# Attention, MLP and a routed expert layer on one core: high halves of the expert weights on ScalarE, another order at the chunk seams

## The chip, the core and the metric

One NeuronCore of a Trainium2 chip runs the whole program. The time is the device time of one execution in microseconds. Five engines run their own instruction lists and meet in semaphores: TensorE (PE), VectorE (DVE), ScalarE (ACT), GpSimd (POOL) and SyncE (SP), which issues most DMAs. An instruction list is worked off in order: a wait in it holds all that stands behind it.

## What is computed

Three layers follow each other. B=4, heads H=8, sequence 576, head width 64, so 2304 tokens of 512 values.

```python
scores = scale * q @ k.T            # causal window of 64
x = softmax(masked scores) @ v      # -> (2304, 512)
h = x @ w_in                        # 512 x 2048
x = (h * sigmoid(1.702 * h)) @ w_out
noisy = x @ w_gate + log1p(exp(x @ w_noise)) * noise   # 8 experts
top2, weights = two largest of noisy, softmax over the two
out[t] = sum over the two of weight * relu(x[t] @ w1[e]) @ w2[e]   # 512 x 1024 x 512
```

## The kernel before

**Products in halves.** Matrices are multiplied as a high part (fp32r, a rounded copy) and a low part (value minus high): each product is three matmuls, high x high, low x high, high x low. So every operand is split by a copy and a subtraction.

**Stages.** Attention runs first. Then the MLP takes NG=6 chunks of TG=384 tokens. A chunk splits its x (split_x: four copies on ScalarE, four subtractions on VectorE), then runs FC=16 iterations c; n = 16g + c counts over all chunks. TensorE's `up` makes a 128-wide slice of h into one of two PSUM banks (12 matmuls), ScalarE makes the sigmoid, VectorE the product `gate`, ScalarE its high part (high_of_gate), VectorE its low part (low_of_gate), TensorE's `down` multiplies the slice with w_out into three y banks (9 matmuls). In order, ScalarE does sigmoid(n), then high_of_gate(n-1); TensorE does up(n), then down(n-2), at c=0 and c=1 too, where the down belongs to the chunk before.

**Routing of chunk g-1 inside chunk g.** copy_y takes the y banks to x2 at c=2; TensorE transposes x2 (turn_x2, from c=4), ScalarE copies the result, TensorE makes logits (from c=6), ScalarE and VectorE soften, choose, assign, weigh and place (c=9 to 14), ranks stands at c=13. Then POOL's scatter_x2(g-1) sends the rows to their experts' regions in DRAM by six indirect DMAs. copy_y of the next chunk waits until they have landed. After the last chunk the routing runs alone, then the routing tables are made (L1007 to L1037) and the experts begin.

**Expert weights.** While the MLP runs, 128 jobs of 256 KB split w1 and w2: SyncE loads raw data into one of four buffers (ej_loaded), POOL multiplies by one into `high` (L530, 3 buffers in xT, one extra) and subtracts (L532), SyncE stores both to split_weights. SyncE's order is load n, store n-2, load n+1, store n-1 and so on; load n waits for the stores of job n-4 to have landed. POOL does 8 jobs, then 24 jobs and a scatter, five times. Ahead of the first load SyncE writes zeros to all of `out` (6 DMAs of 768 KB) and to the pads of the experts' regions.

**Experts.** 40 tiles of 128 rows are used here, of at most SLOTS=43. For each tile, POOL gathers the rows of `out` so far (gather_part), VectorE adds the weighted result (finish, y_sb), and POOL scatters them back (scatter_y). A gather waits only for scatters of earlier experts (the table `settled`) and for its buffer. From tile j = SURE-1 = 35 on, POOL also waits for each scatter to have landed before it goes on (last lines of its block).

Of the kernel before, what the change touches and what calls it, by code (L numbers as in the profile page):

```python
# [11 lines left out]
P = 128  # L12
# [28 lines left out]
QUADS = 2  # L41
GQUADS = (EJOBS // 2 - QUADS) // (NG - 1)
# [9 lines left out]
FAR = 1 << 16  # L52
LG = 2 * E


def after(eng, sem, value):

    if isinstance(value, int) and value <= 0:
        return
    eng.wait_ge(sem, value)  # L60


def build(nc, q, k, v, w_in, w_out, w_gate, w_noise, noise, w1, w2, out):
# [13 lines left out]
    with ctx:  # L77
# [73 lines left out]
        count_to = sbc("count_to", [P, SLOTS])  # L151
        slot_row = sbc("slot_row", [P, SLOTS])
        upto = sbc("upto", [P, E, E], mybir.dt.bfloat16)
        odd = sbc("odd", [P, SLOTS + 1])
# [11 lines left out]
        expert_of = sbc("expert_of", [P, SLOTS], I32)  # L166
        row_of = sbc("row_of", [P, SLOTS], I32)
        ends = sbc("ends", [P, E], I32)
        rows = sbc("rows", [P, SLOTS], I32)
        slot_w = sbc("slot_w", [P, SLOTS])  # L170
        keep = sbc("keep", [P, SLOTS], I32)
        far = sbc("far", [P, SLOTS], I32)
        masked_id = sbc("masked_id", [P, SLOTS], I32)
        passed = sbc("passed", [P, SLOTS, E])
        stepped = sbc("stepped", [P, SLOTS, E])
        past = sbc("past", [P, SLOTS])
        row_f = sbc("row_f", [P, SLOTS])
        first_row = sbc("first_row", [P, SLOTS])
        first_slot = sbc("first_slot", [P, SLOTS])
        settled = sbc("settled", [P, SLOTS], I32)  # L180
        end_row = sbc("end_row", [P, SLOTS])
        valid = sbc("valid", [P, SLOTS])
# [294 lines left out]
        def _(pool):  # L477
# [97 lines left out]
            nc.gpsimd.iota(count_to[:], [[1, SLOTS]], base=0, channel_multiplier=0, allow_small_or_imprecise_dtypes=True).then_inc(slot_consts, 1)  # L575
            nc.gpsimd.iota(slot_row[:], [[P, SLOTS]], base=P, channel_multiplier=0, allow_small_or_imprecise_dtypes=True).then_inc(slot_consts, 1)
            nc.gpsimd.iota(odd[:].rearrange("p (a b) -> p a b", b=2), [[0, (SLOTS + 1) // 2], [1, 2]], base=0, channel_multiplier=0, allow_small_or_imprecise_dtypes=True).then_inc(slot_consts, 1)
# [50 lines left out]
            for j in range(SURE - 1, SLOTS):  # L628
                par = j % 2
                if j < SURE:  # L630
                    gather_part(j, par)
                    scatter_y(j, par)
                    for i in range(2):
                        pool.wait_ge(y_scattered[i], SURE // 2 * 16)
                else:
                    with pool.If(tiles1 > j + 1):
                        gather_part(j, par)
                        scatter_y(j, par)

                        pool.wait_ge(y_scattered[par], (j // 2 + 1) * 16)  # L640

        @block.scalar
        def _(act):
# [70 lines left out]

            def soften(g):
# [11 lines left out]
            def mlp(g, first):  # L727
                split_x(g)
                for c in range(FC):
                    n = g * FC + c  # L730
                    if c == 2 and not first:
# [15 lines left out]
                    if c == 12 and not first:  # L747
# [80 lines left out]
        def _(dve):  # L828
# [140 lines left out]
            def mlp(g, first):  # L969
                split_x(g)  # L970
                if g == 1:
# [47 lines left out]
            then(nc.vector.tensor_tensor(passed[:], end_e[:, None, :].to_broadcast([P, SLOTS, E]),  # L1019
                                         count_to[:, :, None].to_broadcast([P, SLOTS, E]), ALU.is_le))  # L1020
# [352 lines left out]
```

## Time and profile before

| | us |
|---|---|
| median of 3 runs | 1127.85 (1118.88, 1127.85, 1129.74) |
| profiled execution | 1117.89, its span 1116.2 |
| TensorE busy in the span | 998.9 (89%) |
| POOL, VectorE, ScalarE busy | 528.3, 628.7, 448.6 |
| TensorE's mean granted clock | 0.958 |

The profile is of one execution. Idle time of an engine is put down to what released it. The granted clock is a share of full speed: 1.0 is 2.4 GHz and 0.5 is 1.2 GHz. Attention lasts to about 164 us, the MLP from 164 to 598, the last routing to 642, the experts from there to the end.

### The profile page before, as it was taken

What the parts mean: (1) busy time and instruction counts of PE and PEld (TensorE: products, weight loads), DVE (VectorE), ACT (ScalarE), POOL (GpSimd) and SP (SyncE); (2) the same over time, 40 slices, a digit from 0 to 9 for tenths busy, and PEclk for the clock granted to TensorE, in tenths of its full rate; (3) what the DMA queues carried; (4) which work ended last, traced back from release to release, by engine and by line L of the source; (5) the groups of instructions that cost most, each with busy time, mean ns of one, the idle gap of its engine ahead of it and who ended that gap; (6) DMA issues with size and microseconds to landing.
All of it is one profiled execution on the core that took longest, in us unless ns stands there. A gap on an engine that the chain in (4) does not pass through costs nothing.

```text
span 1116.2 us, 21003 instructions
## 1 busy us (share of the span) xinstructions
PE 998.9 (89%) x5376; PEld 851.4 (76%) x5377; DVE 628.7 (56%) x1413; ACT 448.6 (40%) x1088; POOL 528.3 (47%) x511
## 2 busy tenths in 40 slices
PE   5777769999999999999996099999999999999993
PEld 5666659879899898898995078888887888888882
DVE  3777752342433527437353467676767676767671
ACT  4877762222424324233242034343443434343440
POOL 3555553896198889898985202121212121212121
PEclk8999989999999999999997599999999999999997
DMA  7678748998189799898888884586858585859211
GB/s 159 166 186 188 184 118 299 289 292 265 40 262 284 253 287 292 270 295 287 265 269 290 279 260 141 183 252 179 255 168 252 169 258 170 266 166 268 65 58 33
DMA packets 253444, 241.65 MB, mean 216 GB/s; under 512 B 97740, under 2 KB 171468, under 8 KB 253392
## 3 DMA queue, kind: packets, MB, share of 16 engines
q1 hardware_dynamic: 215312, 201.54, 60.4%
q0 software_dynamic: 9280, 28.62, 7.2%
q10 hardware_dynamic: 28800, 10.83, 4.3%
q8 instruction: 29, 0.48, 0.2%
q14 instruction: 23, 0.19, 0.1%
HBM read 148.81 MB, written 94.21 MB: 218 GB/s over the span
## 4 chain that ended last, share of the span: by engine, by line
PE 33%; DMA 17%; issue 13%; DVE 11%; ACT 9%; POOL 7%; ACTq 5%; DVEq 2%; POOLq 1%; SPq 1%
PE bank L1209 14%; PE bank L1224 13%; DMA part<-out,yrow 10%; ACT hq L783 4%; DMA out<-y_sb,yrow 4%; ACTq L766 3%; POOL raw L532 2%; ACT he L790 2%; POOL xT L530 2%; DVE y_sb L1079 2%; DMA w_raw<-moe_w_out 1%; PE bank L1244 1%; DVE hT L1067 1%; PE bank L1146 1%; DVEq L1041 1%
## 5 line engine op out<-in xcount | busy, mean ns | idle before, releaser
L1308 PE MATMUL bank<-W,xe 128*128 x960 | 233.2, 399 | 23.5 <-DVE xe L1054 23.5
L1319 PE MATMUL bank<-W,he 128*128 x960 | 230.5, 395 | 4.1 <-DVE he L1071 4.1
L1308 PEld LDWEIGHTS bank<-W,xe 128*128 128x128 f32 x960 | 182.1, 190 | 67.9 <-issue 23.6
L1209 PE MATMUL bank<-xs,W 128*128 128x384 f32 x1152 | 219.8, 340 | 8.7 <-DVE xs L895 8.6
L1224 PE MATMUL bank<-W,gs 128*128 128x512 f32 x864 | 217.1, 396 | 1.0 <-DVE gs L900 1.0
L1319 PEld LDWEIGHTS bank<-W,he 128*128 128x128 f32 x960 | 179.9, 188 | 49.0 <-issue 5.8
L1209 PEld LDWEIGHTS bank<-xs,W 128*128 128x128 f32 x1152 | 200.3, 189 | 17.0 <-issue 10.3
L1224 PEld LDWEIGHTS bank<-W,gs 128*128 128x128 f32 x864 | 161.7, 188 | 31.9 <-DVE gs L900 1.4
L982 DVE TENSOR_TENSOR gate<-bank,gate 128x384 f32<-128x384 f32 x96 | 53.4, 557 | 232.6 <-ACT gate L736 226.2
L606 POOL DMA_INDIRECT out<-y_sb,yrow x40 | 40.6, 1015 | 291.5 <-DVE y_sb L1079 286.1
L783 ACT ACTIVATE hq<-bank 32x256 f32<-32x256 f32 x320 | 119.7, 374 | 112.7 <-issue 99.9
L736 ACT ACTIVATE gate<-bank 128x384 f32<-128x384 f32 x96 | 47.2, 492 | 281.6 <-PE bank L1209 275.0
L1065 DVE STREAM_TRANSPOSE hT<-bank 32x256 f32<-32x256 f32 x320 | 144.0, 450 | 11.2 <-PE bank L1308 6.2
L532 POOL TENSOR_TENSOR raw<-raw,xT 128x512 fp32r<-128x512 f32 x96 | 129.7, 1351 | 7.5
L530 POOL TENSOR_TENSOR xT<-raw,e_iota 128x512 fp32r<-128x512 f32 x96 | 107.0, 1115 | 38.4 <-DMA raw<-moe_w 37.1
L900 DVE TENSOR_TENSOR gs<-gate,gs 128x384 fp32r<-128x384 f32 x96 | 85.1, 888 | 0.0
L773 ACT ACTIVATE xe<-xr 128x512 fp32r<-128x512 f32 x40 | 25.3, 632 | 139.4 <-DVE xr L1050 136.7
L509 POOL TENSOR_TENSOR prob<-prob,rden 128x384 f32<-128x384 f32 x48 | 39.8, 829 | 74.2 <-DVE rden L852 74.2
L1071 DVE SCALAR_TENSOR_TENSOR he<-hT,he 128x1024 fp32r<-128x1024 f32 x40 | 49.0, 1226 | 45.1 <-ACT he L790 45.1
L661 ACT ACTIVATE prob<-prob,nmx 128x128 f32<-128x128 f32 x144 | 56.1, 391 | 27.8 <-DVE nmx L845 27.6
L560 POOL DMA_INDIRECT x_by_expert<-x,xT x36 | 36.9, 1024 | 58.0 <-issue 37.5
L599 POOL DMA_INDIRECT part<-out,yrow x40 | 42.0, 1050 | 34.9 <-POOL yrow L596 34.9
(148 smaller groups left out, 1031.8 us busy)
## 6 DMA issues: line engine op xcount, KB each, us to landing
W<-split_weights SPq DMA_DIRECT2D x128, 512.0 KB
raw<-moe_w SPq DMA_DIRECT2D x128, 256.0 KB, 3.4
split_weights<-raw SPq DMA_DIRECT2D x128, 256.0 KB, 3.3
split_weights<-xT SPq DMA_DIRECT2D x96, 256.0 KB, 3.1
xg<-x_by_expert ACTq DMA_DIRECT2D x160, 64.0 KB
split_weights<-high SPq DMA_DIRECT2D x32, 256.0 KB
q_raw<-q SPq DMA_DIRECT2D x32, 144.0 KB, 2.9
k_raw<-k SPq DMA_DIRECT2D x32, 144.0 KB, 3.9
```

What stands on the lines that cost most here:

```text
L530: nc.gpsimd.tensor_tensor(high[buf], job_raw[buf], one, ALU.mult).then_inc(ej_high, 1)
L532: nc.gpsimd.tensor_tensor(job_raw[buf].bitcast(F32R), job_raw[buf], high[buf].bitcast(F32), ALU.subtract).then_inc(ej_low, 1)
L661: ins = nc.scalar.activation(prob[m % 3][:, b], prob[m % 3][:, b], ACT.Exp, bias=nmx[:, m % 2, b:b + 1], accum_out=den[:, m % 2, b:b + 1])
L783: ins = nc.scalar.activation(hq[c * Q:(c + 1) * Q, :].rearrange("p (k q i) -> p k q i", q=2, i=Q)[:, :, q], src[q * Q:(q + 1) * Q, :, c], ...
L900: nc.vector.tensor_tensor(gs[c % 2][:, 1], gate[c % 2][:], gs[c % 2][:, 0].bitcast(F32), ALU.subtract).then_inc(g_low, 1)
L982: nc.vector.tensor_tensor(gate[c % 2][:], h_ps[c % 2][:, 0:TG], gate[c % 2][:], ALU.mult).then_inc(gated, 1)
L1065: nc.vector.transpose(dst[c * Q:(c + 1) * Q, :, q], src[q * Q:(q + 1) * Q, :, c])
L1071: nc.vector.scalar_tensor_tensor(out=he[par][:, 1], in0=hT[:], scalar=0.0, in1=he[par][:, 0].bitcast(F32), op0=ALU.max, op1=ALU.subtract). ...
L1209: ins = nc.tensor.matmul(h_ps[c % 2][:, 0:TG], w_in_s[:, wl, d, c * P:(c + 1) * P], xs[:, xl, d], start=(d == 0 and wl + xl == 0), stop=(d ...
L1224: ins = nc.tensor.matmul(y_ps[t][:], gs[c % 2][:, gl, t * P:(t + 1) * P], w_out_s[:, wl, c], start=(c == 0 and gl + wl == 0), stop=(c == F ...
L1308: ins = nc.tensor.matmul(h2_ps[par][:, f * 512:(f + 1) * 512], xe[par][:, xl, d * P:(d + 1) * P], weights(e, wl, d * FE + f * 512), start= ...
L1319: ins = nc.tensor.matmul(ye_ps[par][:], he[par][:, hl, c * P:(c + 1) * P], weights(e, wl, W1COLS + c * DM), start=(c == 0 and wl + hl == 0 ...
```

## The change

- POOL only subtracts (low_of_job). The high parts are copies on ScalarE (high_of_job), put into its MLP iterations by the formula jobs_by: 128 jobs over n=1 to n=93, one or two in each. They stand after high_of_gate and wait for ej_loaded there. c=0 has two from the second chunk on, c=8 two.
- scatter_x2(g) stands on POOL behind the subtractions of the jobs up to c=13 of chunk g+1.
- At a seam TensorE does down(14), up(0), down(15); c=1 has only its up; from c=2 up(c), down(c-2) as before. ScalarE and VectorE finish gate 15 ahead of c=0; high_of_gate(0) comes in c=1, behind copy_y and sigmoid(1).
- copy_y moves from c=2 to c=1, and all of the routing two iterations ahead; place is at c=12.
- The tables get two more columns (TABLE = SLOTS+2); the waits on each scatter at the tail go, and one wait for all scatters stands at the end, its counts read from `settled`.
- SyncE's list is unchanged.

```diff
+def jobs_by(chunk):
+    return min(JOBS, max(0, (chunk - 1) * JOBS // (NG * FC - 3)))
...
-            def split_job(n, buf, count):
-                pool.wait_ge(ej_loaded[buf], count * 16 + 16)
-                one = e_iota[:, None, 1:2].to_broadcast([P, DC, P])
-                nc.gpsimd.tensor_tensor(high[buf], job_raw[buf], one, ALU.mult).then_inc(ej_high, 1)
+            def low_of_job(n):
+                buf = n % 4
                 pool.wait_ge(ej_high, n + 1)
                 nc.gpsimd.tensor_tensor(job_raw[buf].bitcast(F32R), job_raw[buf], high[buf].bitcast(F32), ALU.subtract).then_inc(ej_low, 1)
...
-            pool.wait_ge(xs_low, DC)
-            for i in range(QUADS):
-                for buf in range(4):
-                    split_job(i * 4 + buf, buf, i)
-            for g in range(1, NG):
-                with pool.Fori(QUADS + (g - 1) * GQUADS, QUADS + g * GQUADS) as i:
-                    for buf in range(4):
-                        split_job(i * 4 + buf, buf, i)
-                scatter_x2(g - 1)
+            done = 0
+            for g in range(NG - 1):
+                due = jobs_by((g + 1) * FC + 14)
+                for n in range(done, due):
+                    low_of_job(n)
+                done = due
+                scatter_x2(g)
+            for n in range(done, JOBS):
+                low_of_job(n)
...
                 if j < SURE:
                     gather_part(j, par)
                     scatter_y(j, par)
-                    for i in range(2):
-                        pool.wait_ge(y_scattered[i], SURE // 2 * 16)
                 else:
                     with pool.If(tiles1 > j + 1):
                         gather_part(j, par)
                         scatter_y(j, par)
-                        pool.wait_ge(y_scattered[par], (j // 2 + 1) * 16)
+            for i in range(2):
+                written = pool.value_load(settled[0:1, SLOTS + i:SLOTS + i + 1], min_val=SURE // 2 * 16, max_val=SLOTS * 16)
+                pool.wait_ge(y_scattered[i], written)
+                pool.sem_inc(wait_passed, 1)
...
+            def high_of_job(n):
+                buf = n % 4
+                act.wait_ge(ej_loaded[buf], n // 4 * 16 + 16)
+                nc.scalar.activation(high[buf], job_raw[buf], ACT.Copy).then_inc(ej_high, 1)
...
             def mlp(g, first):
                 split_x(g)
+                if not first:
+                    high_of_gate(g * FC - 1, FC - 1)
                 for c in range(FC):
                     n = g * FC + c
-                    if c == 2 and not first:
+                    if c == 1 and not first:
                         copy_y(g - 1, 0)
                         copy_y(g - 1, 2)
                     act.wait_ge(hidden, n + 1)
                     after(act, g_low, n - 1)
                     nc.scalar.activation(gate[c % 2][:], h_ps[c % 2][:, 0:TG], ACT.Sigmoid, scale=1.702).then_inc(sigmoided, 1)
-                    if not (first and c == 0):
-                        high_of_gate(n - 1, (c - 1) % FC)
-                    if 5 <= c < 5 + GT and not first:
-                        if c == 5:
+                    if c:
+                        high_of_gate(n - 1, c - 1)
+                    for job in range(jobs_by(n), jobs_by(n + 1)):
+                        if job == 0:
+                            act.wait_ge(xs_low, DC)
+                        high_of_job(job)
+                    if 3 <= c < 3 + GT and not first:
+                        if c == 3:
                             act.wait_ge(out_zeroed, ZEROED)
-                        copy_x2T(g - 1, c - 5)
-                    if c == 10 and not first:
+                        copy_x2T(g - 1, c - 3)
+                    if c == 8 and not first:
                         nc.scalar.preload_act_table_set("natural_log_exp_and_others")
                         soften(g - 1)
                         nc.scalar.preload_act_table(ACT.Sigmoid)
-                    if c == 12 and not first:
+                    if c == 10 and not first:
...
             def mlp(g, first):
                 split_x(g)
+                if not first:
+                    low_of_gate(g * FC - 1, FC - 1)
...
                 for c in range(FC):
                     n = g * FC + c
-                    if c == 2 and not first:
+                    if c == 1 and not first:
                         copy_y(g - 1)
                     dve.wait_ge(sigmoided, n + 1)
                     nc.vector.tensor_tensor(gate[c % 2][:], h_ps[c % 2][:, 0:TG], gate[c % 2][:], ALU.mult).then_inc(gated, 1)
-                    if not (first and c == 0):
-                        low_of_gate(n - 1, (c - 1) % FC)
+                    if c:
+                        low_of_gate(n - 1, c - 1)
                     if not first:
+                        if c == 7:
+                            soften(g - 1)
                         if c == 9:
-                            soften(g - 1)
+                            choose(g - 1)
+                        if c == 10:
+                            assign(g - 1)
                         if c == 11:
-                            choose(g - 1)
+                            weigh(g - 1)
                         if c == 12:
-                            assign(g - 1)
-                        if c == 13:
-                            weigh(g - 1)
-                        if c == 14:
                             place(g - 1)
...
             def mlp(g, first):
                 for c in range(FC):
                     n = g * FC + c
+                    if c == 0 and not first:
+                        down(n - 2, FC - 2, g - 1)
                     up(g, c, n)
-                    if not (first and c < 2):
-                        down(n - 2, (c - 2) % FC, g if c >= 2 else g - 1)
+                    if c == 0 and not first:
+                        down(n - 1, FC - 1, g - 1)
+                    if c >= 2:
+                        down(n - 2, c - 2, g)
                     if not first:
+                        if 2 <= c < 2 + GT:
+                            turn_x2(g - 1, c - 2)
                         if 4 <= c < 4 + GT:
-                            turn_x2(g - 1, c - 4)
-                        if 6 <= c < 6 + GT:
-                            logits(g - 1, c - 6)
-                        if c == 13:
+                            logits(g - 1, c - 4)
+                        if c == 11:
                             ranks(g - 1)
```

## Rows read from the trace of the kernel before

**Rows 1.** The windows view: stretch, its length, busy us by engine, PEclk, DMA share, GB/s.

```profile
174.00:180.00 6.00, 6.00 (x31) 5.37 (x30) 1.62 (x4) 1.81 (x4) 0.00 (x0) 1.00 1.03 384
...
232.00:234.00 2.00, 1.78 (x6) 1.67 (x6) 0.24 (x2) 0.40 (x2) 1.92 (x2) 0.50 0.69 216
...
322.00:400.00 78.00, 77.06 (x408) 69.27 (x407) 34.63 (x72) 26.43 (x53) 68.72 (x58) 1.00 0.88 278
```

**Rows 2.** The page's parts 5 and 6: busy, mean ns, idle before; DMA to landing.

```profile
L1209 PE MATMUL bank<-xs,W 128*128 128x384 f32 x1152 | 219.8, 340 | 8.7 <-DVE xs L895 8.6
...
L532 POOL TENSOR_TENSOR raw<-raw,xT 128x512 fp32r<-128x512 f32 x96 | 129.7, 1351 | 7.5
...
L773 ACT ACTIVATE xe<-xr 128x512 fp32r<-128x512 f32 x40 | 25.3, 632 | 139.4 <-DVE xr L1050 136.7
...
raw<-moe_w SPq DMA_DIRECT2D x128, 256.0 KB, 3.4
```

**Rows 3.** The groups view by line: a table load of ScalarE.

```profile
L744 ACT ACT_TABLE_LOAD x4 | 5.1, 1283 | 0.1
```

**Rows 4.** The timeline, start of the MLP: start us, us, engine, line, operation, idle before.

```profile
163.99 6.49 PE L1209 MATMUL bank<-xs,W 128*128 128x384 f32 x36 [1.70 <-DVE xs L895]
...
168.43 0.49 ACT L736 ACTIVATE gate<-bank 128x384 f32<-128x384 f32 x1 [1.59 <-PE bank L1209]
...
170.32 2.26 PE L1224 MATMUL bank<-W,gs 128*128 128x512 f32 x9
...
173.23 9.77 SPq L410 DMA_DIRECT2D raw<-moe_w  x3
...
174.50 2.26 PE L1224 MATMUL bank<-W,gs 128*128 128x512 f32 x9
...
185.87 1.04 POOL L530 TENSOR_TENSOR xT<-raw,e_iota 128x512 fp32r<-128x512 f32 x1 [21.87 <-DMA raw<-moe_w]
```

**Rows 5.** The timeline, TensorE at the seam of chunks 0 and 1.

```profile
228.99 1.28 PE L1209 MATMUL bank<-xs,W 128*128 128x384 f32 x6 [2.08 <-DVE xs L895]
...
233.36 2.61 PE L1224 MATMUL bank<-W,gs 128*128 128x512 f32 x9
```

**Rows 6.** The timeline, first jobs after a scatter: a store, later a load.

```profile
310.62 0.56 SPq L415 DMA_DIRECT2D split_weights<-xT  x1
...
314.92 0.35 SPq L410 DMA_DIRECT2D raw<-moe_w  x1
...
318.82 1.04 POOL L530 TENSOR_TENSOR xT<-raw,e_iota 128x512 fp32r<-128x512 f32 x1 [0.74 <-DMA raw<-moe_w]
...
531.33 0.56 SPq L415 DMA_DIRECT2D split_weights<-xT  x1
...
536.41 0.35 SPq L410 DMA_DIRECT2D raw<-moe_w  x1
```

**Rows 7.** The timeline: a turn inside the MLP, then the end of the MLP.

```profile
546.78 0.60 PE L1237 MATMUL bank<-ident,x 128*128 128x128 f32 x4
...
593.49 4.46 PE L1224 MATMUL bank<-W,gs 128*128 128x512 f32 x18 [0.99 <-DVE gs L900]
...
594.74 1.15 POOL L560 DMA_INDIRECT x_by_expert<-x,xT  x1 [0.15 <-issue]
...
607.76 1.97 PE L1237 MATMUL bank<-ident,x 128*128 128x128 f32 x8 [9.82 <-ACT x L707]
```

**Rows 8.** The chain that ended last: the last scatter's landing.

```profile
601.31 5.42 DMA x_by_expert<-x,xT
```

**Rows 9.** The timeline, the last tiles.

```profile
1092.64 5.87 PE L1319 MATMUL bank<-W,he 128*128 x24 [1.57 <-DVE he L1071]
...
1094.86 1.02 POOL L606 DMA_INDIRECT out<-y_sb,yrow  x1 [5.36 <-issue]
...
1099.85 0.18 POOL L596 COPY yrow<-rows 128x1 int32<-128x1 int32 x1 [3.97 <-issue]
...
1104.40 0.75 DVE L1079 SCALAR_TENSOR_TENSOR y_sb<-bank,slot_w,part 128x512 f32<-128x512 f32 x1 [11.33 <-DMA part<-out,yrow]
```

More of the change, by code:

```diff
@@ L40 @@
 KEPT = 2
-QUADS = 2
-GQUADS = (EJOBS // 2 - QUADS) // (NG - 1)
+JOBS = 2 * EJOBS
 SLOTS = (N * KEPT + E * (P - 1) + E - 1) // P
@@ L52 @@
 FAR = 1 << 16
+TABLE = SLOTS + 2
 LG = 2 * E
@@ L150, in build @@
         to_consts = sbc("to_consts", [P, 2 * TG])
-        count_to = sbc("count_to", [P, SLOTS])
-        slot_row = sbc("slot_row", [P, SLOTS])
+        count_to = sbc("count_to", [P, TABLE])
+        slot_row = sbc("slot_row", [P, TABLE])
         upto = sbc("upto", [P, E, E], mybir.dt.bfloat16)
-        odd = sbc("odd", [P, SLOTS + 1])
+        odd = sbc("odd", [P, TABLE + 1])
         lane = sbc("lane", [P, 1])
@@ L165, in build @@
         hT = sbc("hT", [P, FE])
-        expert_of = sbc("expert_of", [P, SLOTS], I32)
-        row_of = sbc("row_of", [P, SLOTS], I32)
+        expert_of = sbc("expert_of", [P, TABLE], I32)
+        row_of = sbc("row_of", [P, TABLE], I32)
         ends = sbc("ends", [P, E], I32)
[L169 to L182, printed above, removed]
+        rows = sbc("rows", [P, TABLE], I32)
+        slot_w = sbc("slot_w", [P, TABLE])
+        keep = sbc("keep", [P, TABLE], I32)
+        far = sbc("far", [P, TABLE], I32)
+        masked_id = sbc("masked_id", [P, TABLE], I32)
+        passed = sbc("passed", [P, TABLE, E])
+        stepped = sbc("stepped", [P, TABLE, E])
+        past = sbc("past", [P, TABLE])
+        row_f = sbc("row_f", [P, TABLE])
+        first_row = sbc("first_row", [P, TABLE])
+        first_slot = sbc("first_slot", [P, TABLE])
+        settled = sbc("settled", [P, TABLE], I32)
+        end_row = sbc("end_row", [P, TABLE])
+        valid = sbc("valid", [P, TABLE])
         arenas = [[xT[:, d, TG:2 * TG], TG, 0] for d in range(2)]
@@ L562, in scatter_x2 @@
                                                 bounds_check=last_x, oob_is_err=False).then_inc(x2_scattered, 16)
[L564 to L572 removed]
+            done = 0
[7 more added lines that the diff above has]
+                low_of_job(n)
             pool.wait_ge(xs_low, NG * DC)
[L575 to L577 removed]
+            nc.gpsimd.iota(count_to[:], [[1, TABLE]], base=0, channel_multiplier=0, allow_small_or_imprecise_dtypes=True).then_inc(slot_consts, 1)
+            nc.gpsimd.iota(slot_row[:], [[P, TABLE]], base=P, channel_multiplier=0, allow_small_or_imprecise_dtypes=True).then_inc(slot_consts, 1)
+            nc.gpsimd.iota(odd[:].rearrange("p (a b) -> p a b", b=2), [[0, (TABLE + 1) // 2], [1, 2]], base=0, channel_multiplier=0, allow_small_or_imprecise_dtypes=True).then_inc(slot_consts, 1)
             nc.gpsimd.iota(lane[:], [[0, 1]], base=0, channel_multiplier=1, allow_small_or_imprecise_dtypes=True).then_inc(slot_consts, 1)
@@ L1018, in _ @@
             nc.vector.tensor_scalar_add(ends[:], end_e, 1.0)
-            then(nc.vector.tensor_tensor(passed[:], end_e[:, None, :].to_broadcast([P, SLOTS, E]),
-                                         count_to[:, :, None].to_broadcast([P, SLOTS, E]), ALU.is_le))
+            then(nc.vector.tensor_tensor(passed[:], end_e[:, None, :].to_broadcast([P, TABLE, E]),
+                                         count_to[:, :, None].to_broadcast([P, TABLE, E]), ALU.is_le))
             then(nc.vector.reduce_sum(past[:], passed[:], AX.X))
             nc.vector.tensor_single_scalar(expert_of[:], past[:], float(E - 1), ALU.min)
-            then(nc.vector.tensor_tensor(stepped[:], passed[:], tiles_e[:, None, :].to_broadcast([P, SLOTS, E]), ALU.mult))
+            then(nc.vector.tensor_tensor(stepped[:], passed[:], tiles_e[:, None, :].to_broadcast([P, TABLE, E]), ALU.mult))
             nc.vector.scalar_tensor_tensor(out=first_row[:], in0=past[:], scalar=float(CAP), in1=slot_row[:], op0=ALU.mult, op1=ALU.add)
             then(nc.vector.reduce_sum(first_slot[:], stepped[:], AX.X))
-            then(nc.vector.tensor_tensor(settled[:], first_slot[:], odd[:, 0:SLOTS], ALU.add))
+            then(nc.vector.tensor_tensor(settled[:], first_slot[:], odd[:, 0:TABLE], ALU.add))
             then(nc.vector.tensor_single_scalar(settled[:], settled[:], 1, ALU.arith_shift_right))
@@ L1029, in _ @@
             then(nc.vector.scalar_tensor_tensor(out=first_row[:], in0=first_slot[:], scalar=-float(P), in1=first_row[:], op0=ALU.mult, op1=ALU.add))
-            then(nc.vector.tensor_tensor(stepped[:], passed[:], end_step[:, None, :].to_broadcast([P, SLOTS, E]), ALU.mult))
+            then(nc.vector.tensor_tensor(stepped[:], passed[:], end_step[:, None, :].to_broadcast([P, TABLE, E]), ALU.mult))
             then(nc.vector.reduce_sum(end_row[:], stepped[:], AX.X))
```

## The prediction

> **What bounds the kernel now.** I read the busy time by stretch first, then the groups by line, then the timeline at the four places where the first layer's weights, its chunk seams, the hand-over to the experts and the last tile lie. In the middle of the MLP TensorE is busy 77.06 of 78 us [rows 1], so there only what holds TensorE counts. One iteration c is an up and a down: the downs of c=2 and c=3 start at 170.32 and 174.50, 4.18 us apart, 2.09 for each half [rows 4]. ScalarE and VectorE have slack: the down that needs a sigmoid starts 1.9 us after that sigmoid did (168.43 to 170.32) [rows 4], and TensorE gets to it 4.2 us after the sigmoid's up has ended. A sigmoid can be late by about 4.2 - 0.2 - 1.9 = 2.1 us at no cost.
>
> TensorE loses time in three places. At the chunk seams up(0) waits for the split of x: L1209 has 8.7 us of such idle time [rows 2], 1.7 of it at the very start [rows 4], so 7.0 at seams; at the first seam the idle of 2.08 us [rows 5] is followed by a granted clock of 0.50, which is the 1.2 GHz level [rows 1]. That up, begun at 228.99, is followed by its down at 233.36: 4.37 us, less the 2.09 of a normal up and 0.63 of further idle, leaves 1.65, and the down takes 0.35 longer: 2.0 us for the low clock. At the end of the MLP there is 0.99 us, and then 9.82 us until the first transpose [rows 7], because copy_y needs scatter_x2(4) landed, and that stood behind 24 split jobs on POOL. Last, at the tail the gather for tile 39 waits for the scatter of tile 38 [rows 9].
>
> **Gains.** (a) With down(14) ahead of up(0), the split of x has 2.09 us more; the largest first wait was 2.08. All 7.0 + 2.0 go, and the 0.99 too, since POOL's subtractions end at c=13: 10.0 us.
>
> (b) Hand-over. Count from the end of up(13) of the last chunk. ScalarE does sigmoid, gate copy and two jobs (0.2 + 0.9 + 2 x 0.63, [rows 2]) until 2.4; POOL subtracts (1.35 each, [rows 2]) until about 4.4; the six indirect DMAs start 6.6 us from first to last (594.74 to 601.31, [rows 7, 8]), and the last needs 5.42 to land [rows 8]: 16.4, or 15.6 if POOL is not behind with a job. TensorE ends its last down at 2 x 4.18 + 3 x 2.09 = 14.6. The first transpose starts 1.0 after the landing (606.73 to 607.76, [rows 7, 8]). Idle 2.0 to 2.8 in place of 9.82, so 7.4 gained (7.0 to 7.9). Eight transposes took 1.97 there [rows 7], four take 0.60 at full clock [rows 7]; with less idle ahead the clock may hold for this part: 1.0 taken, 0 to 2.5 possible. Together 8.4.
>
> (c) Tail. POOL issues scatter 38 at 1094.86, and copies yrow only at 1099.85 (3.97 us idle); y_sb of tile 39 starts at 1104.40 [rows 9]. Without the wait the copy can follow at once, or 1.05 us later for the register load; TensorE's last down, begun at 1092.64 and 5.87 long [rows 9], is ahead of that gather. 3.4 us (2.9 to 3.9). The final wait at the end moves nothing.
>
> The 128 high parts, 1.1 us each off POOL, were on no path of TensorE apart from (b).
>
> **Losses, first: job 0.** The new ScalarE program puts high_of_job(0) into n=1, with its wait on ej_loaded ahead of sigmoid(2). SyncE's order is not changed: the zeros for out and the pads go first, and in 174 to 180 the DMA share is 1.03 [rows 1]. The first raw loads are issued at 173.23 and job 0's data is there at 185.8: POOL waited 21.87 us for it and started at 185.87 [rows 4]. POOL could wait for free. ScalarE can't: its queue behind job 0 holds sigmoid(2), then high(1), and TensorE needs high(1) for down(1). So ScalarE copies until 186.5, sigmoid(2) starts at 186.55, down(1) at 188.45 instead of 174.50. That is 14.0 us of idle, and the restart is at the low clock, 2.0 us by the first seam. Loads 1 and 2 were issued in the same row and are in by then. 16.0 us; bounds 14 (clock held) to 18.
>
> **Second: the seam after each scatter.** Count from the end of up(14). POOL does low(38) (job numbers of the first such seam), then six indirect DMAs, from -1.0 to 6.7, during which nothing is subtracted. low(39) ends at 8.1 and low(40) at 9.5. SyncE issues load n, store n-2, load n+1, store n-1: so load 42 stands behind store 39 and goes out at 9.6, load 43 needs store 39 landed. After the scatters of before, a load waited for the store of the same buffer 4.3 us (310.62 to 314.92) and 5.1 us (531.33 to 536.41); the load issued at 314.92 was used at 318.82, after a wait: 3.9 [rows 6]; the median of all is 3.4 [rows 2]. So load 42 is in at 13.1 and load 43 at 8.2 + 5.0 + 3.4 = 16.6 (16.0 to 17.1). By the formula of jobs_by both fall into c=0 of the next chunk (31*128/93 = 42 for n=32, 32*128/93 = 44 for n=33; 22 more at each later seam), and ScalarE wants them at 11.2 and 11.8. Behind them in its queue: copy_y twice (1.1), sigmoid(1), high(0). Job 43's copy ends at 17.3, sigmoid(1) starts at 18.5, down(0) 1.9 later at 20.4. TensorE is at down(0) at 4.18 + 6 x 2.09 = 16.7: 3.7 us of idle (3.0 to 4.2), four times (the seams behind scatters 0 to 3). The nearest row for the clock is the first seam, where 2.7 us of idle within 5.3 cost 2.0: taken here too, between 0 and 2.0. Four times 5.7 = 22.8 (12 to 25).
>
> For a DMA of 256 KB there is another figure. The Trainium skill ("DMA: Bandwidth & Descriptors", Anatomy of one DMA) fits 2.0 us plus bytes over 436 GB/s, which is 2.6 us (an estimate by that page, and for the software path). The trace doesn't agree: its median for such a load is 3.4 [rows 2]. By that page, with 0.7 for the second store's issue, job 43 would be in at 14.1, the seam's stall would be 1.2 and the whole sum, with no clock loss, +0.5.
>
> **Third: c=8.** It holds two jobs (1.3 us) and soften with two table loads of 1.28 [rows 3] and two small activations, some 3.1. Sigmoid, gate copy and these end 5.5 after the up; the next sigmoid was due at 4.4, so it is 1.1 late, 1.7 with a short load wait: within the 2.1 of slack unless VectorE is slow as well. 0 to 1.8 per chunk; 0.3 taken, 1.5 in all.
>
> ScalarE's load is no bound: 1.84 us of each 4.18 in the mean. The DMA pace is none either: 0.77 MB per 3.04 us is 252 GB/s, and 278 were carried in 322 to 400 [rows 1]. The two wider columns of the tables and the longer straight-line programs are taken as 0.
>
> **Sum.** 16.0 + 22.8 + 1.5 - 10.0 - 8.4 - 3.4 = +18.5 us. Against the profiled execution (1117.89 us; span 1116.2) that is 1136.4. That execution is at the low end: the runs are 1118.88, 1127.85 and 1129.74. I put the sum on the middle of the four, 1123.6: **1142 us**, 1.6% more.
>
> **Rivals.** (1) Seams stall, but the clock holds: 3.7 us in one piece is less time than the 5.3 us over which the first seam's trouble was spread, with TensorE busy before and after. 4 x 2.0 less: +10.5, 1134. (2) ScalarE is late inside the chunk too: at c=8 the full 1.8 each time, 9 instead of 1.5. Speaks for it: two jobs and two table loads in one iteration. +26, 1150. (3) Short seams: a store is back as soon as the median load, 3.4, so that job 43 is in at 15.0; stall 2.1, no clock loss. Speaks for it: right after a scatter the DMA queues are empty. Against it: the 4.3 to 5.1 of [rows 6] were measured at just that point. 4 x 3.6 less: +4.1, 1128. (4) The other side, faster: ScalarE's waits on loads never reach TensorE, as the change needs. Place: ej_loaded in high_of_job; all losses but c=8 vanish, -20.3, 1103. It decides once TensorE's stalls by jobs stay under about 9 us in all; the start alone has 14 by [rows 4], so for this job 0's load would have to land by 173.
>
> **How the numbers follow.** About 1% is what a measurement of this kernel tells from no change, here 11 us. Forecast 0.42; clock holds at seams 0.20; c=8 0.13; short seams 0.15; never waits 0.10. Slower by over 1%: forecast, c=8 and half of the clock case, 0.65. Within 1%: short seams and the other half, 0.25. Faster: 0.10. The range leaves out the last case alone and part of its neighbours: from short seams with job 0's stall at its lower bound, on a low run (1118.9 + 2.1 = 1121), to c=8 on the high run (1129.7 + 26 = 1156). The likeliest case's own range is 1130 to 1150.
>
> **What the profile after would show.** Right: on ScalarE one wait for raw of some 16 us near 170, TensorE idle about 14 us from 174.5; at four seams TensorE idle 3 to 4 us ahead of down(0), put down to gs or ScalarE, with ScalarE waiting on raw before; no wait of up(0) for xs; idle before the first transpose at the hand-over 2 to 3 us; last y_sb 3.4 us sooner after the last down. Wrong: sigmoid(2) on time (then the losses are not there), or the seam waits gone although POOL scatters for 7.7 us, or waits of TensorE inside chunks, which would mean the pace of the loads bounds.

## The result, and the profile after

| | before | after |
|---|---|---|
| median, side by side on one chip (14 runs each) | 1123.78 us (1116.85 to 1129.74) | 1132.47 us (1129.36 to 1145.01) |
| profiled execution | 1117.89 | 1132.05, its span 1130.2 |
| TensorE busy | 998.9 | 1006.7 |
| POOL, VectorE, ScalarE busy | 528.3, 628.7, 448.6 | 378.3, 605.8, 517.3 |
| TensorE's mean granted clock | 0.958 | 0.953 |

The ratio is 1.009, 95% interval 1.0059 to 1.0121. The changed kernel is slower, by about one per cent. The rows below are of the kernel after unless a sentence says otherwise; L1225 is up, L1240 down, L909 VectorE's split of x, L914 its low_of_gate, L721 high_of_job, L534 low_of_job.

From the page's part 5, the groups (busy, mean ns | idle before, releaser):

```profile
L1240 PE MATMUL bank<-W,gs 128*128 128x512 f32 x864 | 221.1, 402 | 19.8 <-DVE gs L914 19.8
...
L1225 PE MATMUL bank<-xs,W 128*128 128x384 f32 x1152 | 221.2, 343 | 6.9 <-DVE xs L909 6.9
...
L998 DVE TENSOR_TENSOR gate<-bank,gate 128x384 f32<-128x384 f32 x96 | 53.6, 558 | 273.9 <-ACT gate L746 255.8
...
L914 DVE TENSOR_TENSOR gs<-gate,gs 128x384 fp32r<-128x384 f32 x96 | 60.0, 625 | 1.2 <-ACT gs L702 1.2
```

TensorE's idle time in the MLP is 26.7 us here (19.8 ahead of downs, 6.9 ahead of ups). Before, it was 9.7: 8.7 ahead of ups [rows 2] and 0.99 ahead of the last downs [rows 7]. The timeline shows where it lies. First the start of the MLP, ScalarE and TensorE (start us, us, engine, line, operation, idle before):

```profile
186.60 0.63 ACT L721 ACTIVATE xT<-raw 128x512 fp32r<-128x512 f32 x1 [14.22 <-DMA raw<-moe_w]
...
164.81 8.71 PE L1225 MATMUL bank<-xs,W 128*128 128x384 f32 x36 [1.70 <-DVE xs L909]
...
189.05 4.21 PE L1240 MATMUL bank<-W,gs 128*128 128x512 f32 x9 [11.35 <-DVE gs L914]
...
195.36 2.26 PE L1240 MATMUL bank<-W,gs 128*128 128x512 f32 x9
```

ScalarE waits for job 0's raw data until 186.60, and down(1) starts at 189.05, 24.24 us after the MLP's first up, where it was 10.51 in [rows 4]: 13.7 later. The next down follows after 6.31 instead of 4.18, which is 2.1 of low clock (granted 0.50 in the window of 189 to 193). That is 15.9 us.

Then the four seams behind a scatter, TensorE:

```profile
319.35 3.76 PE L1225 MATMUL bank<-xs,W 128*128 128x384 f32 x12 [2.58 <-DVE xs L909]
...
394.34 3.72 PE L1240 MATMUL bank<-W,gs 128*128 128x512 f32 x9 [4.21 <-DVE gs L914]
...
471.89 2.32 PE L1225 MATMUL bank<-xs,W 128*128 128x384 f32 x12 [2.58 <-DVE xs L909]
...
545.32 3.81 PE L1240 MATMUL bank<-W,gs 128*128 128x512 f32 x9 [4.22 <-DVE gs L914]
```

The idle time is 2.58 + 4.21 + 2.58 + 4.22 = 13.6 us. At three of the four the group behind it takes 3.7 to 3.8 us instead of 2.25: the low clock. At the first, the next up starts at 325.17, 1.64 us later than two normal halves of 2.09 behind 319.35 would put it; three times that is 4.9. In all 18.5 us. The windows view of 319 to 323 has the clock at 0.60, against 1.00 just ahead:

```profile
315.00:319.00 4.00, 1.77 (x8) 1.11 (x6) 4.00 (x1) 1.11 (x3) 3.77 (x4) 1.00 0.60 208
319.00:323.00 4.00, 3.65 (x13) 3.69 (x14) 2.08 (x5) 0.00 (x0) 0.00 (x0) 0.60 0.98 294
```

The waits of 2.58 us stand ahead of up(0). Those of 4.21 and 4.22 us stand ahead of down(14), which comes before up(0) in the new order.

**What holds TensorE there is VectorE, and what holds VectorE goes with POOL.** VectorE and POOL at the first two of these seams:

```profile
314.49 6.12 DVE L909 TENSOR_TENSOR xs<-xT,xs 128x384 fp32r<-128x384 f32 x4 [0.32 <-issue]
...
313.82 1.20 POOL L562 DMA_INDIRECT x_by_expert<-x,xT  x1 [0.30 <-issue]
315.02 1.32 POOL L534 TENSOR_TENSOR raw<-raw,high 128x512 fp32r<-128x512 f32 x1
316.28 2.50 POOL L534 TENSOR_TENSOR raw<-raw,xT 128x512 fp32r<-128x512 f32 x2
...
389.07 0.56 DVE L998 TENSOR_TENSOR gate<-bank,gate 128x384 f32<-128x384 f32 x1 [3.63 <-issue]
389.54 4.74 DVE L914 TENSOR_TENSOR gs<-gate,gs 128x384 fp32r<-128x384 f32 x1
...
390.14 2.50 POOL L534 TENSOR_TENSOR raw<-raw,xT 128x512 fp32r<-128x512 f32 x2
392.59 1.27 POOL L534 TENSOR_TENSOR raw<-raw,high 128x512 fp32r<-128x512 f32 x1
```

While POOL ran the indirect DMAs of the scatter, three jobs (39 to 41 at the first seam) piled up, and it subtracts them back to back: 315.02 to 318.78, and 390.14 to 393.86. The one subtraction of VectorE that meets this burst ends only 0.42 us after it, at 319.20 and 394.28. By the view of line L909, at the first seam that is one operation of 4714 ns among four whose median is 546. At the fourth seam low_of_gate begins only at 541.94, inside the burst of 541.11 to 544.84, lasts 3.33 us and again ends 0.43 us behind it. Whether it is the split of x or low_of_gate depends on which is due then. The product at L998, which reads one operand from PSUM, has the mean 558 ns (559 at most) against 557 before, when POOL was busier; the low part, with both operands in SBUF, went from 888 to 625.

In before, POOL's instructions never held VectorE that long although it had more of them: no operation of the split or of low_of_gate lasted over 1.65 us. POOL's subtraction waited for its own multiplication, and the trace has a break of 0.1 us between the two. VectorE at the seam of chunks 0 and 1, and POOL beside it, of before:

```profile
225.86 1.45 DVE L900 TENSOR_TENSOR gs<-gate,gs 128x384 fp32r<-128x384 f32 x1
227.23 4.95 DVE L895 TENSOR_TENSOR xs<-xT,xs 128x384 fp32r<-128x384 f32 x4
...
225.85 1.05 POOL L530 TENSOR_TENSOR high<-raw,e_iota 128x512 fp32r<-128x512 f32 x1
226.97 1.46 POOL L532 TENSOR_TENSOR raw<-raw,high 128x512 fp32r<-128x512 f32 x1
```

POOL is idle from 226.90 to 226.97. The low part at 225.86 ended at 227.31, 0.41 us behind POOL's multiplication, although POOL's next subtraction had begun: the break let it in. Of VectorE's four split operations behind it the longest took 1.63 us and the shortest 0.55 (the view of L895): none was held for more than about one instruction of POOL.

**The hand-over and the tail** gained what they should, nearly:

```profile
625.54 1.09 PE L1253 MATMUL bank<-ident,x 128*128 128x128 f32 x8 [3.24 <-ACT x L709]
...
1110.81 5.87 PE L1339 MATMUL bank<-W,he 128*128 x24 [1.56 <-DVE he L1087]
...
1113.02 1.02 POOL L608 DMA_INDIRECT out<-y_sb,yrow  x1 [8.35 <-issue]
1114.05 0.20 POOL L598 COPY yrow<-rows 128x1 int32<-128x1 int32 x1
...
1118.62 0.75 DVE L1095 SCALAR_TENSOR_TENSOR y_sb<-bank,slot_w,part 128x512 f32<-128x512 f32 x1 [7.39 <-issue]
```

The first transpose waits 3.24 us instead of 9.82 [rows 7]. The copy of yrow now follows the scatter at once, and y_sb starts 7.81 us after the last down instead of 11.76 [rows 9]; from that down to the span's end it is 19.39 instead of 23.56.

**The account, profile to profile:** attention +0.8, first up to last down +23.5, idle ahead of the transposes -6.6, last routing -0.2, experts +0.6, tail -4.2: +13.9 of the 14.0 us by which the span grew. In first up to last down, job 0 and the seams have +15.9 and +18.5, so some 10.9 us were gained there. The medians differ by only 8.7: the profiled execution of before lay 5.9 us under its own median, that of after 0.4 under its own. Which stage makes before's executions differ among themselves is not known.

### The profile page after: what moved, and what is told of

The parts are those of the page before. It is cut to its first block, busy times and chain, and to the rows that moved or that the text cites. A ratio compares the mean times of both kernels' runs of the same rounds, so it can differ in the third digit from the quotient of the medians.

```text
span 1130.2 us, 20791 instructions
## 1 busy us (share of the span) xinstructions
PE 1006.7 (89%) x5376; PEld 858.6 (76%) x5377; DVE 605.8 (54%) x1413; ACT 517.3 (46%) x1216; POOL 378.3 (33%) x383
## 4 chain that ended last, share of the span: by engine, by line
PE 62%; DMA 9%; issue 8%; DVE 7%; ACT 6%; POOL 2%; ACTq 2%; SPq 1%; DVEq 1%; POOLq 0%
PE bank L1225 16%; PE bank L1240 15%; PE bank L1339 13%; PE bank L1328 13%; DMA part<-out,yrow 3%; ACT hq L797 2%; PE bank L1260 2%; DMA out<-y_sb,yrow 1%; PE bank L1162 1%; ACTq L780 1%; DMA w_raw<-moe_w_in 1%; DMA w_raw<-moe_w_out 1%; DMA raw<-moe_w 1%; DMA x_by_expert<-x,xT 1%; DVE gs L914 1%
## 5 line engine op out<-in xcount | busy, mean ns | idle before, releaser
L1240 PE MATMUL bank<-W,gs 128*128 128x512 f32 x864 | 221.1, 402 | 19.8 <-DVE gs L914 19.8
L1225 PE MATMUL bank<-xs,W 128*128 128x384 f32 x1152 | 221.2, 343 | 6.9 <-DVE xs L909 6.9
L1225 PEld LDWEIGHTS bank<-xs,W 128*128 128x128 f32 x1152 | 204.0, 192 | 13.1 <-issue 7.8
L1240 PEld LDWEIGHTS bank<-W,gs 128*128 128x128 f32 x864 | 164.6, 192 | 52.6 <-DVE gs L914 21.0
L998 DVE TENSOR_TENSOR gate<-bank,gate 128x384 f32<-128x384 f32 x96 | 53.6, 558 | 273.9 <-ACT gate L746 255.8
L534 POOL TENSOR_TENSOR raw<-raw,xT 128x512 fp32r<-128x512 f32 x96 | 123.1, 1290 | 202.7 <-ACT xT L721 202.6
L1081 DVE STREAM_TRANSPOSE hT<-bank 32x256 f32<-32x256 f32 x320 | 144.0, 450 | 10.9 <-PE bank L1328 5.9
L721 ACT ACTIVATE xT<-raw 128x512 fp32r<-128x512 f32 x96 | 58.5, 623 | 18.2 <-DMA raw<-moe_w 18.2
L914 DVE TENSOR_TENSOR gs<-gate,gs 128x384 fp32r<-128x384 f32 x96 | 60.0, 625 | 1.2 <-ACT gs L702 1.2
L534 POOL TENSOR_TENSOR raw<-raw,high 128x512 fp32r<-128x512 f32 x32 | 41.3, 1291 | 49.4 <-ACT high L721 49.4
L804 ACT ACTIVATE he<-hT 128x1024 fp32r<-128x1024 f32 x40 | 42.5, 1061 | 33.6 <-DVE hT L1083 32.1
```

The lines of the kernel that those rows point to most:

```text
L721: nc.scalar.activation(high[buf], job_raw[buf], ACT.Copy).then_inc(ej_high, 1)
L914: nc.vector.tensor_tensor(gs[c % 2][:, 1], gate[c % 2][:], gs[c % 2][:, 0].bitcast(F32), ALU.subtract).then_inc(g_low, 1)
L998: nc.vector.tensor_tensor(gate[c % 2][:], h_ps[c % 2][:, 0:TG], gate[c % 2][:], ALU.mult).then_inc(gated, 1)
L1081: nc.vector.transpose(dst[c * Q:(c + 1) * Q, :, q], src[q * Q:(q + 1) * Q, :, c])
L1225: ins = nc.tensor.matmul(h_ps[c % 2][:, 0:TG], w_in_s[:, wl, d, c * P:(c + 1) * P], xs[:, xl, d], start=(d == 0 and wl + xl == 0), stop=(d ...
L1240: ins = nc.tensor.matmul(y_ps[t][:], gs[c % 2][:, gl, t * P:(t + 1) * P], w_out_s[:, wl, c], start=(c == 0 and gl + wl == 0), stop=(c == F ...
```

## Experiments

Every run was timed against before on the same chip; ratios are to before, with their 95% intervals. Edits are on the changed kernel unless said. Idle times are those of each kernel's profiled execution.

**late: the jobs begin at n=6 instead of n=1.** It tests the start term.

```diff
-    return min(JOBS, max(0, (chunk - 1) * JOBS // (NG * FC - 3)))
+    return min(JOBS, max(0, (chunk - 6) * JOBS // (NG * FC - 8)))
```

> The changed kernel, with the 128 jobs given out over n=6 to n=93 in place of n=1 to n=93; nothing else moves. Theory: ScalarE's wait for job 0 holds TensorE at the start of the MLP, and that costs about 13.7 us of delay of down(1) plus 2.1 us of low clock after it; then TensorE has no idle time above 1 us in the first chunk and the time falls by 14 to 16 us against the changed kernel (about 1117, ratio to before 0.994 to 0.997). Rival: the first loads are late whatever ScalarE does, or the denser later jobs (one more in every 20 iterations) make new waits in the chunks: then 8 us or less are won.

Measured 1117.39 us, ratio 0.9967 (0.9941 to 0.9992). No idle time is left in the first chunk but the 1.70 us at its start; the seams stay (2.58, 4.06, 2.60, 2.58 us). From 1.009 to 0.9967 is 13.8 us, for a term of 15.9 in the trace. The 4.06 has another wait in it: the jobs now stand closer together, and ScalarE waited 2.84 us for raw data, until 379.71, just ahead of its copies for the split.

**c0shift: no job in c=0.** From the second chunk on, c=0 to 5 get 0, 1, 2, 2, 2, 1 jobs in place of 2, 1, 1, 2, 1, 1. If ScalarE's wait for load 43 made the stall, as predicted, it goes.

```diff
-                    for job in range(jobs_by(n), jobs_by(n + 1)):
+                    jobs = range(jobs_by(n), jobs_by(n + 1))
+                    if not first and c < 6:
+                        lo = jobs_by(g * FC)
+                        jobs = range(lo + (0, 0, 1, 3, 5, 7)[c], lo + (0, 1, 3, 5, 7, 8)[c])
+                    for job in jobs:
```

> The changed kernel, with the two jobs of c=0 moved behind c=1 and c=2 in chunks 1 to 5 (0, 1, 2, 2, 2, 1 jobs in c=0 to 5). Theory of the prediction (ScalarE waits at c=0 for load 43, which stands behind the scatter): the seam idle of TensorE, 2.6, 4.2, 2.6, 4.2 us in the trace after, goes, and the time falls by 13 us or more. Rival (VectorE's subtraction at the seam is held by the three subtractions that POOL does back to back after a scatter, 6.1 us for four split operations or 4.7 us for one of the gate): the seam idle stays at 2.6 to 4.2, the time moves by less than 2 us.

Measured 1128.79 us, ratio 1.0081 (1.0053 to 1.0109): nothing gained that stands out of the noise. All four seams of this kernel have 2.57 or 2.58 us ahead of up(0); the first and the last:

```profile
313.78 3.54 PE L1229 MATMUL bank<-xs,W 128*128 128x384 f32 x12 [2.57 <-DVE xs L913]
...
540.14 3.74 PE L1229 MATMUL bank<-xs,W 128*128 128x384 f32 x12 [2.58 <-DVE xs L913]
```

**lowwait: POOL waits, behind the scatter, for the split of x before its backlog.** It takes the overlap of POOL and VectorE away.

```diff
                 scatter_x2(g)
+                if g < NG - 2:
+                    pool.wait_ge(xs_low, (g + 3) * DC)
```

> The changed kernel, with one wait added on POOL: after each scatter (not the last) the subtractions go on only when the next chunk's x is split. Rival theory (VectorE held by POOL): VectorE's four split operations take 2.0 us in all and no gate subtraction above 1.4 us at seams; up(0) does not wait for xs; but the loads 42 and 43 come about 2 us later, so that ScalarE waits on raw in c=0 and down(0) is 2 to 4 us late at four seams. Time against the changed kernel within 4 us. Theory of the prediction alone (loads bound the seam, VectorE does not): seam idle grows by 2 us each, 8 us slower or more.

Measured 1130.08 us, ratio 1.0089 (1.0059 to 1.0119). The wait for xs is gone and another stands in its place. TensorE, then ScalarE, of this kernel at the first such seam:

```profile
326.24 2.94 PE L1242 MATMUL bank<-W,gs 128*128 128x512 f32 x9 [2.68 <-DVE gs L916]
...
320.94 0.63 ACT L723 ACTIVATE xT<-raw 128x512 fp32r<-128x512 f32 x1 [3.10 <-DMA raw<-moe_w]
323.15 0.63 ACT L723 ACTIVATE high<-raw 128x512 fp32r<-128x512 f32 x1 [1.58 <-DMA raw<-moe_w]
```

The four are 2.68, 3.40, 2.69 and 3.80 us, ahead of down(0), with ScalarE waiting on raw in c=0: the stall that had been predicted, in its place. But the edit makes a part of it. POOL now stands still ahead of its backlog at each of the four seams, and the stores and loads behind it come later by as much:

```profile
314.98 1.53 POOL L534 TENSOR_TENSOR raw<-raw,high 128x512 fp32r<-128x512 f32 x1 [1.52 <-DVE xs L911]
```

Less these 1.5 us, an estimate for the stall by the loads alone is 1.2, 1.9, 1.2 and 2.3 us, where 3.7 each had been predicted.

**both: c0shift and lowwait together.**

> The last two together: no jobs at c=0, and POOL's subtractions after a scatter wait for the split of x. If VectorE held by POOL is the first limit of the seam and the load of job 43 the second, only the two together clear it: seam idle under 1 us each, no low clock there, 15 to 18 us less than the changed kernel. If one of the two edits alone already gives that, the other theory falls. If a third limit is there, the seam idle stays above 1 us.

Measured 1111.14 us, ratio 0.9909 (0.9884 to 0.9934). No seam has any idle time. Either edit alone gave 1 us or nothing, the two give 1.009 - 0.9909 = 0.0181, 20.3 us, beside the 18.5 counted in the trace. Two limits lay one behind the other: VectorE held by POOL, and, once POOL waits, ScalarE behind the loads.

**gap: behind each of the three backlog subtractions POOL sets a small spare tile to zero** (the line that allocates it is left out here). Does an instruction that reads nothing let VectorE in?

```diff
                     low_of_job(n)
+                    if g and n - done < 3:
+                        nc.gpsimd.memset(spare[:, (g - 1) * 3 + n - done], 0.0)
```

> The changed kernel, with a memset of 12 columns on POOL behind each of the three subtractions that follow a scatter. It reads nothing. Theory A: VectorE's subtraction gets its turn only when POOL has a moment without a reading instruction, and in a burst there is none; with the memsets one of VectorE's operations is held by one subtraction (1.3 us), not by three (3.9 to 4.2 us), so the longest split operation falls below 2 us and seam idle drops to 2 us or less. Theory B: VectorE is held by POOL's queue as a whole, or waits for all of the burst for another reason (it has to be idle): no change, 3 to 4.7 us for the longest operation, seam idle 2.6 and 4.2 us as after.

Measured 1134.94 us (two runs), ratio 1.0116 (1.0078 to 1.0154). VectorE and POOL of this kernel:

```profile
313.26 4.90 DVE L917 TENSOR_TENSOR gs<-gate,gs 128x384 fp32r<-128x384 f32 x1
...
313.93 1.29 POOL L535 TENSOR_TENSOR raw<-raw,high 128x512 fp32r<-128x512 f32 x1
315.14 0.13 POOL L573 MEMSET spare<- 128x12 f32 x1
315.21 1.27 POOL L535 TENSOR_TENSOR raw<-raw,xT 128x512 fp32r<-128x512 f32 x1
```

No: the operation of VectorE is held over the whole burst, zeroing and all.

**drain: POOL waits for its own last subtraction before each of the three.** This puts back the break that before had.

```diff
                 for n in range(done, due):
+                    if g and n - done < 3:
+                        pool.wait_ge(ej_low, n)
                     low_of_job(n)
```

> Edit: on the changed kernel, POOL waits, before each of the three backlog subtractions behind a scatter, for the semaphore of its own subtraction before, so that one is complete before the next begins. Theory (the wait is VectorE's, held as long as POOL's subtractions follow one another without a break, and a break lets it in): no operation of VectorE with two inputs in SBUF at the four seams lasts over some 2 us, where 3.33 to 6.12 for one or four stood; TensorE's idle there falls from 2.58, 4.21, 2.58 and 4.22 us to under 1 each, about -10 us of idle and -4 of low clock, ratio 0.995 to 1.000 instead of 1.009. Rival (it is the sum of POOL's work that costs, or a break of this length is not seen by VectorE): the four waits stay within 0.5 us of 2.6 and 4.2 us and the ratio stays at 1.007 to 1.012. Second rival (with the first limit gone ScalarE's wait on the loads behind the scatter shows, as with the early wait on POOL): waits of 2 to 4 us on VectorE's low part of the gate's result, with ScalarE idle on raw before them, ratio 1.004 to 1.010.

Measured 1123.67 us, ratio 1.0011 (0.9989 to 1.0033), some 9 us better than the changed kernel. VectorE and POOL of this kernel at the first such seam:

```profile
315.24 5.85 DVE L911 TENSOR_TENSOR xs<-xT,xs 128x384 fp32r<-128x384 f32 x4 [0.32 <-ACT xs L699]
...
315.78 1.31 POOL L534 TENSOR_TENSOR raw<-raw,high 128x512 fp32r<-128x512 f32 x1
317.18 3.03 POOL L534 TENSOR_TENSOR raw<-raw,xT 128x512 fp32r<-128x512 f32 x2
```

From 317.09 to 317.18 POOL does nothing, and that is enough: the four operations of VectorE take 2283, 1631, 1623 and 545 ns instead of one 4714 and three of 546. The first ends at 317.52. The sum is nearly the same, but the first parts come early enough for up(0) to start, and TensorE's waits are 0.70 and 0.75 us at each seam (at the third 0.15 more), no longer 2.6 or 4.2. That is above the 1 us per seam that I expected, one operation lasts over 2 us, and the ratio lies just above the expected 0.995 to 1.000; direction and cause hold. The loads made no stall here: c=0 has its two jobs as in the changed kernel, and no down(0) waits at any of the four seams; ScalarE's own waits for raw data there are 0.73 and 0.65 us at the second and the fourth.

**late_c0_drain: late, c0shift and drain.**

> Edit: the jobs spread over the later part of the MLP, those of the chunks behind a scatter moved to the chunks after, and POOL waiting for its own last subtraction before each of the three of the backlog. Theory (breaks let VectorE in): no seam with over 1 us of idle, as with the early wait in POOL in place of the breaks, which gave 1104.0 us and ratio 0.983; expected 1101 to 1107 us, ratio 0.980 to 0.987. Rival (breaks do nothing): four waits of 2.6 us on VectorE's split as in the run that moved the jobs alone, some 10 to 14 us more, ratio 0.992 to 0.998.

Measured 1111.67 us, ratio 0.9917 (0.9888 to 0.9945). That lies between the two expectations. TensorE's waits at the seams are 1.46, 2.59, 1.65 and 1.45 us, so breaks do less than keeping POOL away. At the second seam a wait of ScalarE for raw data (2.11 us, to 376.18) ahead of the copies for the split has a part in it, as in late.

**late_both: late, c0shift and lowwait.** In this kernel and in late_c0_drain the last number of c0shift's table is `jobs_by(g * FC + 6) - lo` in place of 8, as late's formula gives 9 jobs in some chunks.

> The changed kernel with the three edits tried before: jobs over n=6 to n=93, none in c=0, POOL waits for the split of x behind a scatter. If the two causes (job 0's wait, the seam) are independent, their gains add: 14 us and 17 to 19 us off the changed kernel, about 1100, ratio to before 0.98. If the seam edit only worked because job 0's stall had shifted the work against the loads, less than 25 us in all.

Measured 1104.02 us, ratio 0.9829 (0.9795 to 0.9864): the lowest median of this study, ahead of both; its interval meets that of late_inter below. In the MLP only 1.70 us of idle remain beside the 1.70 at its start:

```profile
375.13 2.33 PE L1231 MATMUL bank<-xs,W 128*128 128x384 f32 x12 [1.70 <-DVE xs L915]
```

The two gains, 0.0123 and 0.0181, would give 0.9786 if they added in full; it is 0.0043 (4.8 us) short of that, which four ratios with intervals of 0.0025 to 0.0035 to either side do not tell from nothing. Against before it is 19.2 us faster, for gains of 21.8 (10.0 + 8.4 + 3.4) in the prediction.

**late_inter: late, and the backlog's three subtractions go one each between the last scatter DMAs.** Another way to break the burst.

```diff
-            def scatter_x2(g):
+            def scatter_x2(g, between=()):
...
+                        if between and at in between:
+                            for n in between[at]:
+                                low_of_job(n)
...
-                scatter_x2(g)
+                extra = range(due, min(JOBS, due + 3))
+                scatter_x2(g, {at: [n] for at, n in zip((3, 4, 5), extra)})
+                done = due + len(extra)
```

> Two edits on the changed kernel: jobs over n=6 to n=93, and on POOL the three subtractions that follow a scatter are put between its last three indirect DMAs, so no burst of three stands at the seam and the stores of those jobs go out up to 4 us earlier. Theory (VectorE held by the burst first, load of the second job of c=0 next): both causes shrink together, seam idle under 1 us at each of four seams, no wait for job 0. Time 1100 to 1106, ratio to before 0.98 to 0.985. Rival: a single subtraction on POOL is enough to hold the split of x, or the scatter gets so much longer that copy_y waits for it: seam idle of 1 to 2.5 us stays, 1108 to 1115.

Measured 1106.43 us, ratio 0.9865 (0.9841 to 0.9888), 0.0102 (11.4 us) under late, between the two times that were expected. The seams have 0.58, 2.83, 1.07 and 0.82 us where late has 11.8 in all. The 2.83 is not VectorE held by a burst: ScalarE waited 2.80 us for raw data, until 373.04, ahead of its copies for the split.

**tail: before, with the change's two table columns and its waits at the tail alone.** The lines that go are shown; the wider tables and the one wait at the end are as in the change:

```diff
-                    for i in range(2):
-                        pool.wait_ge(y_scattered[i], SURE // 2 * 16)
...
-                        pool.wait_ge(y_scattered[par], (j // 2 + 1) * 16)
```

> The kernel before with the tail's part of the change alone: the tables two columns wider, no waits on each scatter from tile 35 on, one wait at the end. Expected from the trace after (last down's start to the end 19.4 us against 23.6): 4 us faster, ratio 0.996, and y_sb of the last tile within 8 us of the last down's start. Rival: the gain in the trace after was an accident of that execution, or needs the routing's other timing: ratio 1.0.

Measured 1115.55 us, ratio 0.9947 (0.9917 to 0.9976), which is 3 to 9 us less. The trace has the last y_sb 7.9 us after the last down, as the changed kernel has it.

The hand-over was not tried alone: its gain is read from the trace.

## Why the prediction was right, and where it was not

It said 1142 us and slower; 1132.47 came, inside the range, and slower by 0.6 to 1.2%, at the edge of what the text called slower. The rise was 8.7 us where 18.5 had been added up. The start, the hand-over and the tail were right in mechanism. At the seams the mechanism was wrong, and that its size came near is luck.

- **Job 0: right.** Predicted 14.0 of idle and 2.0 of clock, measured 13.7 and 2.1. The first three ups happened to run at a lower clock (granted 0.71 in 165 to 173; 8.71 instead of 6.49 us), so only 11.35 of it shows as idle. late confirms it with 13.8.
- **Seams behind scatters: size near, cause wrong.** 22.8 us predicted, 18.5 measured. The failing step is "VectorE is ready, ScalarE waits for load 43". The count of POOL's work was right (six DMAs, then a backlog), but it was followed only through what waits for POOL's results, not through what runs beside them. The text's test "no wait of up(0) for xs" failed at two of four seams, and at the other two the wait was ahead of down(14); none was ahead of down(0). c0shift, alone, refutes the named cause. lowwait shows that it stood one step behind, at an estimated 1.2 to 2.3 us without that edit's own delay, for a predicted 3.7; drain, where up(0) is late by only some 1.5 us, shows no such stall at all. One input was mis-sized: the load of the same buffer went out 3.1 us after the first store at the seam (316.50 to 319.61), and 3.7, 3.1 and 3.7 at the others, not the 5.0 taken from the 4.3 and 5.1 of [rows 6]. With 3.1 and 3.7 the prediction's own chain gives a stall of 1.8 or 2.4.
- **Clock at the seams:** taken at 2.0 four times, it was about 1.6 three times. The rival in which the clock holds was wrong at three, right at one.
- **Seams before (a): right.** No idle time at the seam of chunks 0 and 1, none ahead of the last downs; "both" has none at any seam. 10.0 predicted, some 10.9 by the account above.
- **Hand-over (b):** 7.4 of idle predicted, 6.6 measured; of the 1.0 for the clock 0.2 came, since the routing behind took 34.8 us instead of 35.0.
- **Tail (c):** 3.4 predicted, 4.2 measured.
- **c=8:** 1.5 predicted, no idle time there. This rival is out, as is "never waits". (The pace of the loads in that section is 259 GB/s for 768 KB in 3.04 us, not 252; it stays below the 278 that it is compared with.)
- **The base:** +18.5 was predicted and the profiles differ by 14.2; the medians differ by 8.7. Of the miss of 9.5 us 4.3 are the size of the terms, and most of the rest is that before's profiled execution lay low among its runs, so that terms read from it came out larger than the medians bear out. In which stage is open.

"Short seams" gave 1128, nearer to the result than the forecast. Its quicker store is in the trace (3.1 and 3.7 us), but it is not what held TensorE.

## What to carry to other kernels

When work is moved off an engine that shares a path to memory with another, look at how its instructions now follow one another: fewer but without breaks can hold a neighbour longer than more with breaks. Put such bursts where the neighbour's next result is not on the critical path. And when an edit that removes a wait gains nothing, read which wait ends last now, before its cause is given up: here each of two fixes gave nothing alone and both together gave 20 us. Ask, too, how much of the new wait the fix made itself: lowwait held POOL for 1.5 us at each seam, and the loads behind POOL came that much later. A first load that lies behind a big transfer should be waited for only by an engine that has nothing else to do.

## What the runs showed of the hardware

An operation of VectorE with two inputs in SBUF that meets subtractions of POOL does not wait for one of them: it was held until three in a row were done (4.71 us for an operation of 0.55), and with short memsets between them it still was (4.90 us). A break of 0.1 us in POOL's list lets one operation through. The operation that has one input in PSUM never stretched (558 ns, 559 at most). Indirect DMAs of POOL alone held nothing: in the changed kernel low_of_gate began at 313.61, met the one of 313.82 to 315.02 and took 0.55 us. When a hold begins the records do not show well: in the changed kernel the held operations begin up to 0.6 us ahead of the burst's first subtraction (389.54 against 390.14), where one of 0.55 us would have been about done. The Trainium skill ("SBUF — State Buffer", Who interferes with whom) says that a VectorE instruction with two SBUF inputs contends with a GpSimd instruction that reads SBUF. The same page of the Trainium skill (SBUF: two separate sides) says that whichever of the two starts first gets the shared ports for the whole instruction. The trace agrees on which operations are held. It goes further on how long: one instruction of POOL is 1.3 us here, the measured hold was a whole burst, and the memset, which reads nothing, did not end it. Whether POOL's next instruction asks for the ports before it has let go of them, or VectorE sees a release late, no run here tells.
